# Rolling the middle of an unrolled mixture-of-experts stage into hardware loops, on one Trainium2 core

## The chip, the cores and the metric

The kernel runs on one core of a Trainium2 chip. The metric is the device time of one execution in microseconds. A core has five instruction streams that meet only at semaphores: TensorE (PE: matmuls, with its weight loads listed as PEld), VectorE (DVE), ScalarE (ACT), GpSimd (POOL) and SyncE (SP), which here issues the DMAs. Each engine reads its own program. Where the program is straight, every instruction is executed once; where it has a loop, the engine jumps back to code that it has had before and wait values are computed from the loop's counter. A difference within 0.2% of the time can't be told from no change.

## What is computed

Three layers in float32, on 4 x 576 = 2304 tokens of width 512.

```
# attention through 32 packed queries for each of 4 x 8 heads
p_packed = softmax(p k^T / 8) v            # 32 x 64
x = softmax(q p_packed^T / 8) p_packed     # 576 x 64, heads put side by side: 2304 x 512

# 8 experts, dense, weights from 8 Sinkhorn steps on exp(x @ w_gate)
out = 0
for e in range(8):
    h = maximum(x @ w1[e], 0)              # 2304 x 1024
    out += P[:, e:e+1] * (h @ w2[e])       # 2304 x 512

# MLP
r = maximum(out @ w_in, 0)                 # 2304 x 2048
result = (s * r * r + b) @ w_out
```

## The kernel before

Every float32 factor is split in two parts, hi and lo, and a product is three matmul passes (hi hi, hi lo, lo hi), in `three_passes`. The time has three stages. Attention comes first, with the order of its work written out by hand for each engine. The experts come next, from about 90 to 1310 us, and the MLP last.

**Groups.** The hidden units of the experts are worked in groups of 256 (`FG`), four groups to an expert (`PER_EXPERT`), 32 groups in all (`MOE_GROUPS`). Groups 0 to 4 are done plainly. Groups 5 (`SEVEN`) to 31 use a scheme with seven products in place of eight: since x is a product of small attention weights `a` and packed values, `x @ w1` is done as `a @ g`, where `g` (the packed values times w1) is a small matrix made for each group, and the 2 x 2 block product `a @ g` of one batch is done with seven block products and some sums.

**One group on each engine** goes in four steps (`UNITS7`), one for each batch of tokens:
- PE: `unit_of_seven`, seven products of three passes with 288 columns, into four PSUM banks; then `outputs`, four or five token tiles of `h @ w2` of 128 x 512, six matmuls each, into two PSUM banks in turn; after the first of these tiles `fill`, four matmuls of 256 columns toward `g` of a later group. Before tile t PE waits for `acc_done`, that is for DVE to have read tile t - 2's bank. Inside a unit PE waits for `p1_copied` (ACT has copied the first product) and twice for `joined` (DVE has made the sums U2 and U3), because the banks of those sums are written again.
- ACT: `unit_of_seven`, the copy of the first product, then two ReLUs that write `h_hi`; and `shift_fill`, eight small copies that place `g` in `g_raw`.
- DVE: `joins`, seven additions; then `output` for each tile, which waits for `y_full` and adds the tile times the token's gate to `acc`; and two `lo_of_joined`, which write `h_lo`. U2 and U3 are the first two additions.
- POOL: `split_heads` and `split_w2` split the weights that have been loaded into hi and lo; `blocks_of_batch`, once for each batch, makes the seven blocks of the next group's `g`.
- SP: loads the weights of each group, in a loop over the experts, four groups to a turn (`with sp.Fori(1, E) as e`).

All engines run groups 5 to 31 from straight code: PE, ACT and POOL through `groups_of_seven`, DVE through a loop of its own over `group_of_seven`, which is given the operation that adds a tile (`shared(e)`, with the column of the gate that belongs to expert e).

**The MLP** is 8 groups of 256 hidden units in five chunks of tokens each (`mlp_steps`). The first two groups are straight code, and the other six are a loop on PE, ACT and DVE, three turns of two groups:

```
with eng.Fori(1, MLP_GROUPS // 2) as mp:
    for par in range(2):
        for c in range(MC):
            step(mp * 2 + par, par, c)
```

POOL has a loop of the same three turns. In such a loop a wait such as `pe.wait_ge(acc_done, m * TILES + ...)` compares with a value that the engine makes from the counter with a register instruction.

Of the kernel before, what the change touches and what calls it, by code (L numbers as in the profile page):

```python
# [10 lines left out]
ds = bass.ds  # L11
# [7 lines left out]
def attention_moe_mlp(nc, q, k, v, p, w_gate, w1, w2, w_in, w_out, s_, b_, out):  # L19
# [3 lines left out]
    E, FE = w1.shape[0], w1.shape[2]  # L23
# [24 lines left out]
    PER_EXPERT = FE // FG  # L48
    MOE_GROUPS, MLP_GROUPS = E * PER_EXPERT, FM // FG
# [6 lines left out]
    with ExitStack() as ctx:  # L56
# [3 lines left out]
        def sb(name, shape, dt=F32, scope=ctx):  # L60
            return scope.enter_context(nc.sbuf_tensor(name, shape, dt))
# [15 lines left out]
        gate = sb("gate", [P, TILES, E])  # L77
# [222 lines left out]
        SEVEN = FIRST  # L300
# [21 lines left out]
        def hidden_count(g, b, f):  # L322
            return g * GC + (b * FC + f)

        def groups_of_seven(eng, group):
            for g in range(SEVEN, MOE_GROUPS):
                group(g, g % 2)

# [1 line left out]
        MCHUNKS = [(at, min(BANK, N - at)) for at in range(0, N, BANK)]  # L331
        MC = len(MCHUNKS)
        assert MC % 2 == 1 and all(n % P == 0 for _, n in MCHUNKS)

        def slot_of(par, c):
# [59 lines left out]
        def pieces_of_tile(t):  # L395
            found = []
            for b in range(B):
                for c, (_, n) in enumerate(CHUNKS):
                    for r in range(2):
                        at = first_col(b, c) + r * n  # L400
                        lo, hi = max(at, t * P), min(at + n, (t + 1) * P)
                        if lo < hi:
                            found.append((b, c, r, lo - at, hi - at, lo - t * P))
            return found
# [7 lines left out]
        def scores2_of(b, c):  # L412
            at = s2_bank(b, c) * BANK + BANK - H * NPACK
            _, rows, groups = PARTS[c]
            return PS[0:rows, at:at + groups * NPACK].rearrange("s (h n) -> s h n", n=NPACK)
# [176 lines left out]
        def _(pool):  # L592
# [157 lines left out]
            def group_of_seven(g, par):  # L750
# [5 lines left out]
                if ahead:  # L756
# [8 lines left out]
                    blocks_of_batch(g + 1, 1 - par, 3)  # L765

            groups_of_seven(pool, group_of_seven)
            split_in(MOE_GROUPS + 1, 1)
            pool.wait_ge(y_full, MOE_GROUPS * TILES)
# [10 lines left out]
        def _(act):  # L780
# [268 lines left out]
            for j in range(2):  # L1049
                shift_fill(SEVEN + 1, 0, j)  # L1050
            groups_of_seven(act, group_of_seven)

            def turned(some):
# [29 lines left out]
        def _(dve):  # L1083
# [138 lines left out]
            def output(g, tile, add):  # L1222
                dve.wait_ge(y_full, g * TILES + (tile + 1))
                add(acc[:, tile, :], bank(YB + tile % 2), tile).then_inc(acc_done, 1)
# [6 lines left out]

            def shared(e):
                def add(dst, y, tile):
                    share = gate[:, tile, e:e + 1]
                    return nc.vector.scalar_tensor_tensor(out=dst, in0=y, scalar=share, in1=dst,  # L1235
                                                          op0=ALU.mult, op1=ALU.add)
                return add
# [163 lines left out]
            def unit_and_tiles(g, b, g_out, tiles, add, between=None):  # L1401
                joins(g, b)
                for n, t in enumerate(tiles):
                    output(g_out, t, add)
                    if n < FC:
                        lo_of_joined(g, b, 1 - n)
                    if between:
                        between(t)

            def group_of_seven(g, add, between=None):  # L1410
                last = isinstance(g, int) and g == MOE_GROUPS - 1
                for n, (u, half, t0, t1) in enumerate(UNITS7):
                    of = 1 if n >= 2 else 0
                    tiles = range(of * UT + t0, of * UT + t1)
                    if n == 3 and last:
                        for t in tiles:
                            output(g, t, add)
                            between(t)
                    else:
                        unit_and_tiles(g + 1 if n == 3 else g, 2 * u + half, g, tiles, add, between if n >= 2 else None)  # L1420
# [8 lines left out]
            expert_group(UNSCALED, scaled_then_shared, ahead_of_seven)  # L1429
            for n in range(1, PER_EXPERT):  # L1430
                group_of_seven(UNSCALED + n, shared(1))
            for g in range(SEVEN + PER_EXPERT - 1, MOE_GROUPS - 1):
                group_of_seven(g, shared(g // PER_EXPERT))

            def inputs_lo(step):
# [51 lines left out]
        def _(pe):  # L1488
# [511 lines left out]

            eight_to_seven(SEVEN - 1, 0)
            groups_of_seven(pe, group_of_seven)

            def mlp_hidden(m, par, c, f):
# [61 lines left out]
```

## Time and profile before

| | |
|---|---|
| median of 3 runs | 1712.21 us (1711.3 to 1714.53) |
| profiled execution | 1711.3 us; its span 1709.5 us |
| PE busy | 1700.5 us |
| DVE, POOL, ACT busy | 1195.6, 1029.8 and 734.9 us |
| mean granted TensorE clock | 1.0 of full speed |
| instructions | 27307 |

The span is from the first to the last instruction of the profiled execution; the time has 1.8 us more around it. Busy shares are means over stages with different limits, so the views of a stretch say more than the page. Register, branch and semaphore instructions aren't shown in the views; they are part of the count of instructions. Instructions themselves are fetched by DMA, and the profile lists the packets of that as queues of the kind "instruction": q8 carries packets of 16 KB for PE, q14 packets of 8 KB for the others.

### The profile page before, as it was taken

Reading aid. Unit: us, or ns where it says so; the run is one execution under the profiler, and the core shown is the slowest. Engines: PE = TensorE matmul, PEld = TensorE weight load, DVE = VectorE, ACT = ScalarE, POOL = GpSimd, SP = SyncE. Lnnn points to the kernel's source line nnn. Section 1 sums busy time; section 2 is a strip of 40 time slices with the busy share of each in tenths; the row PEclk is TensorE's granted clock in tenths of the full one; section 3 lists DMA queues with packets and bytes.
Section 4 is the critical chain, followed back from the end, with each engine's and each line's share of the span. In section 5 each row is a group of like instructions: output and inputs, shape, how many; then the busy total and the mean of one; then the engine's idle time right before and its main releaser. Section 6 shows DMA issues by size and latency. Waiting matters only on the chain.

```text
span 1709.5 us, 27307 instructions
## 1 busy us (share of the span) xinstructions
PE 1700.5 (99%) x9933; PEld 1474.6 (86%) x9933; DVE 1195.6 (70%) x2119; ACT 734.9 (43%) x1672; POOL 1029.8 (60%) x1200
## 2 busy tenths in 40 slices
PE   9999999999999999999999999999999999999999
PEld 7888888888888888888888888888888888888887
DVE  4846646787777777787778787878787555555555
ACT  5644466454545444544445444545433222222222
POOL 1266669988888888788888877888872010111100
PEclk9999999999999999999999999999999999999999
DMA  9431111111112211111121111112101000000003
GB/s 281 122 81 38 50 38 25 38 49 39 38 38 51 49 38 38 50 38 38 38 62 38 38 43 45 38 38 48 40 25 38 13 20 18 25 25 25 0 0 110
DMA packets 71847, 79.71 MB, mean 47 GB/s; under 512 B 7984, under 2 KB 59184, under 8 KB 71728
## 3 DMA queue, kind: packets, MB, share of 16 engines
q1 hardware_dynamic: 71728, 78.15, 17.1%
q8 instruction: 72, 1.18, 0.3%
q14 instruction: 47, 0.39, 0.1%
HBM read 73.42 MB, written 4.72 MB: 46 GB/s over the span
## 4 chain that ended last, share of the span: by engine, by line
PE 96%; POOL 2%; ACT 1%; DMA 0%; issue 0%; DVE 0%; SPq 0%; POOLq 0%; DVEq 0%
PE PS L1490 94%; PE PS L1510 2%; ACT g_raw L782 1%; PE PS L1724 0%; DMA k_raw<-k_dram 0%; POOL w_lo L606 0%; POOL span_late L695 0%; POOL recombined L679 0%; POOL sums_of_a L687 0%; POOL w_lo L621 0%; POOL w_hi L604 0%; POOL span_late L697 0%; POOL a_parts L699 0%; ACT acc L812 0%; POOL g_slots L727 0%
## 5 line engine op out<-in xcount | busy, mean ns | idle before, releaser
L1490 PE MATMUL PS<-w_hi,h_hi 128*128 128x512 f32 x1440 | 564.6, 392 | 0.6 <-DVE acc L1235 0.6
L1490 PE MATMUL PS<-w_lo,h_hi 128*128 128x512 f32 x1440 | 563.1, 391 | 0.0
L1490 PE MATMUL PS<-w_hi,h_lo 128*128 128x512 f32 x1440 | 560.4, 389 | 0.0
L1235 DVE SCALAR_TENSOR_TENSOR acc<-PS,gate,acc 128x512 f32<-128x512 f32 x504 | 378.4, 751 | 178.9 <-PE PS L1490 178.9
L782 ACT ACTIVATE g_raw<-PS 32x256 f32<-32x256 f32 x992 | 372.0, 375 | 12.3 <-PE PS L1490 0.4
L1490 PEld LDWEIGHTS PS<-w_hi,h_lo 128*128 128x128 f32 x1440 | 270.5, 188 | 58.3
L1490 PEld LDWEIGHTS PS<-w_hi,h_hi 128*128 128x128 f32 x1440 | 270.8, 188 | 50.5 <-DVE acc L1235 0.8
L1490 PEld LDWEIGHTS PS<-w_lo,h_hi 128*128 128x128 f32 x1440 | 270.9, 188 | 46.9
L998 ACT ACTIVATE h_hi<-PS 128x576 fp32r<-128x576 f32 x216 | 128.9, 649 | 303.5 <-DVE PS L1371 303.5
L1490 PE MATMUL PS<-a_parts,g_slots 128*128 128x288 f32 x1296 | 225.1, 295 | 0.1
L604 POOL CAST w_hi<-stage 128x1024 fp32r<-128x1024 f32 (+1 forms) x78 | 76.6, 982 | 238.9 <-PE PS L1490 218.1
L1490 PEld LDWEIGHTS PS<-a_parts,g_slots 128*128 128x128 f32 x1296 | 195.7, 188 | 9.6 <-POOL g_slots L727 0.5
L1371 DVE TENSOR_TENSOR PS<-PS,snaps 128x288 f32<-128x288 f32 x432 | 177.3, 456 | 0.1
L1371 DVE TENSOR_TENSOR snaps<-PS,snaps 128x288 f32<-128x288 f32 x324 | 148.4, 458 | 38.7 <-ACT snaps L782 15.5
L606 POOL TENSOR_TENSOR w_lo<-stage,w_hi 128x1024 fp32r<-128x1024 f32 (+1 forms) x78 | 170.0, 2179 | 6.2
L1490 PE MATMUL PS<-sums_of_a,g_slots 128*128 128x288 f32 x972 | 164.1, 295 | 0.6 <-ACT snaps L782 0.6
L1230 DVE TENSOR_TENSOR acc<-PS,acc 128x512 f32<-128x512 f32 x180 | 124.2, 690 | 56.8 <-PE PS L1490 55.6
L1394 DVE SCALAR_TENSOR_TENSOR h_lo<-PS,h_hi 128x576 fp32r<-128x576 f32 x216 | 161.6, 748 | 0.0
L727 POOL TENSOR_TENSOR g_slots<-g_sums,g_slots 128x512 fp32r<-128x512 f32 x108 | 139.8, 1295 | 8.5
L1490 PEld LDWEIGHTS PS<-sums_of_a,g_slots 128*128 128x128 f32 x972 | 140.7, 188 | 0.8 <-ACT snaps L782 0.8
L782 ACT ACTIVATE snaps<-PS 128x288 f32<-128x288 f32 x108 | 44.4, 411 | 221.4 <-PE PS L1490 221.4
L1067 ACT ACTIVATE mlp_f<-PS 128x512 f32<-128x512 f32 (+1 forms) x80 | 44.4, 556 | 220.0 <-PE PS L1490 220.0
(158 smaller groups left out, 2155.8 us busy)
## 6 DMA issues: line engine op xcount, KB each, us to landing
stage<-moe_w_dram SPq DMA_DIRECT2D x96, 512.0 KB, 4.9
k_raw<-k_dram SPq DMA_DIRECT2D x8, 512.0 KB, 6.4
q_raw<-q_dram SPq DMA_DIRECT2D x8, 512.0 KB, 5.2
v_raw<-v_dram SPq DMA_DIRECT2D x8, 512.0 KB, 6.8
stage<-moe_w_in_dram SPq DMA_DIRECT2D x16, 256.0 KB, 3.0
stage<-moe_w_out_dram SPq DMA_DIRECT2D x8, 512.0 KB, 3.6
out_dram<-acc SPq DMA_DIRECT2D x16, 256.0 KB, 2.3
p_twice<-p_dram SPq DMA_DIRECT2D x8, 64.0 KB, 4.2
```

Source lines behind the costliest of these rows:

```text
L604: nc.gpsimd.tensor_copy(hi, src).then_inc(w1_ready, 1)
L606: nc.gpsimd.tensor_tensor(lo, src, hi.bitcast(F32), ALU.subtract).then_inc(w1_ready, 1)
L727: nc.gpsimd.tensor_tensor(lo[:, GS1:BLOCKS, :], g_sums[:], hi[:, GS1:BLOCKS, :].bitcast(F32), ALU.subtract).then_inc(g_split, 1)
L782: return nc.scalar.activation(dst, src, ACT.Copy)
L998: nc.scalar.activation(h_hi[:, f, b % 2 * S:(b % 2 + 1) * S].rearrange("p (i n) -> p i n", i=2), bank(HB + 2 * f, 2 * BANK).rearrange("p ( ...
L1067: nc.scalar.activation(mlp_f[:, slot, f, 0:n], bank(HB + 2 * slot + f, n), ACT.Relu).then_inc(relu_ready, 1)
L1230: return nc.vector.tensor_tensor(dst, y, dst, ALU.add)
L1235: return nc.vector.scalar_tensor_tensor(out=dst, in0=y, scalar=share, in1=dst, op0=ALU.mult, op1=ALU.add)
L1371: nc.vector.tensor_tensor(dst, bank(at, SPAN), term, ALU.add).then_inc(joined, 1)
L1394: nc.vector.scalar_tensor_tensor(out=h_lo[:, f, cols].rearrange("p (i n) -> p i n", i=2), in0=bank(HB + 2 * f, 2 * BANK).rearrange("p (i n ...
L1490: return nc.tensor.matmul(dst, lhsT, rhs, start=start, stop=stop)
L1510: last = nc.tensor.transpose(bank(unit_bank(unit))[0:m_, c0:c0 + k_], src, ident[0:k_, 0:k_])
```

## The change

`groups_of_seven`, which PE, ACT and POOL use, did groups 5 to 31 in straight code. It now does groups 5 to 28 in a loop of 12 turns with two groups each, and 29 to 31 in straight code. DVE did groups 5 to 30 in straight code ahead of a last, special one. It still does groups 5 to 7 so; groups 8 to 27 are a loop over experts 2 to 6, with four groups to a turn; 28 to 30 are straight again. For the loop, the gate's column is taken with `ds(e, 1)`, an offset that may come from a register.

```
         def groups_of_seven(eng, group):
-            for g in range(SEVEN, MOE_GROUPS):
+            with eng.Fori((SEVEN + 1) // 2, MOE_GROUPS // 2 - 1) as gp:
+                group(gp * 2 - 1, 1)
+                group(gp * 2, 0)
+            for g in range(MOE_GROUPS - 3, MOE_GROUPS):
                 group(g, g % 2)
...
             def shared(e):
                 def add(dst, y, tile):
-                    share = gate[:, tile, e:e + 1]
+                    share = gate[:, tile, ds(e, 1)]
...
             for n in range(1, PER_EXPERT):
                 group_of_seven(UNSCALED + n, shared(1))
-            for g in range(SEVEN + PER_EXPERT - 1, MOE_GROUPS - 1):
-                group_of_seven(g, shared(g // PER_EXPERT))
+            with dve.Fori(2, E - 1) as e:
+                for n in range(PER_EXPERT):
+                    group_of_seven(e * PER_EXPERT + n, shared(e))
+            for n in range(PER_EXPERT - 1):
+                group_of_seven(MOE_GROUPS - PER_EXPERT + n, shared(E - 1))
```

## Rows read from the trace of the kernel before

**Rows 1.** The page: span, busy time of each engine, granted clock.
```profile
span 1709.5 us, 27307 instructions
...
PE 1700.5 (99%) x9933; PEld 1474.6 (86%) x9933; DVE 1195.6 (70%) x2119; ACT 734.9 (43%) x1672; POOL 1029.8 (60%) x1200
...
PEclk9999999999999999999999999999999999999999
```

**Rows 2.** Windows, two in the expert stage, one in the MLP.
```profile
core 0: us, PE busy (x) PEld busy (x) DVE busy (x) ACT busy (x) POOL busy (x), PEclk, DMA share, GB/s
292.00:692.00 400.00, 399.45 (x2202) 352.30 (x2201) 317.71 (x574) 192.12 (x465) 332.02 (x412) 1.00 0.17 42
692.00:1092.00 400.00, 400.00 (x2204) 353.04 (x2203) 318.23 (x572) 194.62 (x472) 328.01 (x408) 1.00 0.18 43
...
1505.00:1603.00 98.00, 98.00 (x457) 82.10 (x456) 52.89 (x76) 24.58 (x40) 15.08 (x13) 1.00 0.07 21
```

**Rows 3.** The chain that ended last: start us, us, what.
```profile
539.26 754.45 PE PS L1490 x4153
```

**Rows 4.** Groups of DVE instructions on the page: busy us, mean ns, idle before.
```profile
L1235 DVE SCALAR_TENSOR_TENSOR acc<-PS,gate,acc 128x512 f32<-128x512 f32 x504 | 378.4, 751 | 178.9 <-PE PS L1490 178.9
...
L1371 DVE TENSOR_TENSOR snaps<-PS,snaps 128x288 f32<-128x288 f32 x324 | 148.4, 458 | 38.7 <-ACT snaps L782 15.5
```

**Rows 5.** Waits in 692 to 1092 us: us in total, times, longest.
```profile
ACT h_hi L998 <- DVE PS L1371: 121.1, 43, 3.0
...
DVE acc L1235 <- PE PS L1490: 67.2, 148, 0.6
POOL g_slots L715 <- ACT g_raw L782: 37.9, 10, 4.1
...
PEld PS L1490 <- DVE snaps L1371: 0.2, 1, 0.2
```

**Rows 6.** Timeline of DVE, last output of a step and the joins of the next.
```profile
801.13 0.75 DVE L1235 SCALAR_TENSOR_TENSOR acc<-PS,gate,acc 128x512 f32<-128x512 f32 x1 [0.61 <-PE PS L1490]
802.03 1.02 DVE L1371 TENSOR_TENSOR snaps<-PS,snaps 128x288 f32<-128x288 f32 x2 [0.15 <-ACT snaps L782]
...
803.89 1.18 DVE L1371 TENSOR_TENSOR PS<-PS,snaps 128x288 f32<-128x288 f32 x3
```

**Rows 7.** Timeline of PE's weight loads in the same unit.
```profile
802.39 0.45 PEld L1490 LDWEIGHTS PS<-sums_of_a,g_slots 128*128 128x128 f32 x3
802.78 0.86 PEld L1490 LDWEIGHTS PS<-a_parts,g_slots 128*128 128x128 f32 x6
803.59 0.19 PEld L1490 LDWEIGHTS PS<-w_hi,h_hi 128*128 128x128 f32 x1
```

**Rows 8.** Instruction fetches in 692 to 1092 us: packets, MB, share.
```profile
q8 instruction: 17, 0.28, 0.3%
q14 instruction: 13, 0.11, 0.1%
```

**Rows 9.** All DMA queues in 1505 to 1603 us, the MLP loop's second turn.
```profile
DMA packets 1632, 2.10 MB, mean 21 GB/s; under 512 B 96, under 2 KB 1120, under 8 KB 1632
...
q1 hardware_dynamic: 1632, 2.10, 6.7%
```

**Rows 10.** Instruction fetches in 1407 to 1505 us, the MLP loop's first turn.
```profile
q8 instruction: 4, 0.07, 0.3%
q14 instruction: 1, 0.01, 0.0%
```

**Rows 11.** DMA issues on the page: count, KB each, median us to landing.
```profile
stage<-moe_w_in_dram SPq DMA_DIRECT2D x16, 256.0 KB, 3.0
...
out_dram<-acc SPq DMA_DIRECT2D x8, 64.0 KB, 1.7
...
s_and_b<-moe_b_dram SPq DMA_DIRECT2D x1, 0.5 KB, 8.2
```

## The prediction

> **What bounds the kernel now.** I read the page first: the span is 1709.5 us, PE is busy for 1700.5 us of it, and the granted clock is at full speed throughout (the 2.4 GHz level) [rows 1]. So nearly all of the time is matmul time. Next I read the windows of the stage that the change rewrites (the groups of seven products, about 292 to 1294 us): PE is busy 399.45 and 400.00 us of two windows of 400 us [rows 2]. The chain that ended last agrees: one unbroken piece of 754.45 us with 4153 matmuls [rows 3]. By the code a group has 18 output tiles x 6, 28 products x 3 and 4 fills x 4 = 208 matmuls, so 4153 are 20 groups of 37.7 us. The reader should take two things from this. There is nothing to win in this stage: PE never stops, and the change removes no matmul. And there is no reserve: what stops PE once is added to the end.
>
> Behind PE stand engines that are fairly full. In the second window DVE is busy 318 of 400 us, POOL 328, ACT 195 [rows 2]. By the table of waits DVE idles 67.2 us there before outputs, waiting for PE, ACT 121.1 us for DVE, POOL 37.9 us for ACT's copies; PE's weight loads waited 0.2 us for a DVE join, once [rows 5]. This last row is small but telling: the join is the place where PE nearly touches DVE. The timeline shows how nearly. DVE starts its last output at 801.13, takes 0.75, and starts the first join of the next unit at 802.03 [rows 6]. A join takes 0.46 us [rows 4], so the first is done at 802.49. The product that needs it has its first weight load at 802.78 [rows 7]: 0.29 us to spare. The second join ends at 803.05 (802.03 + 1.02 for two); the product that needs it is three loads behind 802.78, at about 803.19 (6 loads end at 803.64): 0.14 us to spare.
>
> **The change part by part.** It removes no arithmetic, transfer or wait. It rolls 24 of 27 groups into a loop of 12 turns of two groups on PE, ACT and POOL, and 20 groups into a loop of 5 turns of four groups on DVE. It adds three things.
>
> 1. *Wait values.* Every wait in a loop compares with a value made from the counter, so a register instruction stands ahead of each distinct value. Counted from the code, a group has about 43 such values on PE, 54 on DVE, 17 on ACT, 33 on POOL. Cost: the kernel's last stage is such a loop already (two blocks of 256 hidden units a turn). There PE is busy 98.00 of 98.00 us, with a back edge inside the window [rows 2]. So on PE the values and the branch cost nothing that shows: they run under queued matmuls (0.23 us each there, 0.13 us each for the narrow products). On DVE an output takes 0.75 us and its values are made under the instruction before it. Where two joins follow each other in 0.37 us (three take 1.18 us [rows 6]) one or two values must fit; no row prices one, so I bound it: 0 below; above, if every one of 24 x 4 units lost 0.1 us beyond the 0.14 to spare, +10 us. I take 0.
>
> 2. *The gate's column* becomes a register address in 360 outputs. PE needs the result of a tile two tiles later. A tile is 6 x 0.227 = 1.36 us, an output 0.75 us, and DVE idles 0.45 to 0.61 us before most of them (67.2/148, and 0.61 in the timeline) [rows 5, 6]. Address work ahead of the wait is hidden by that idle time; if the cover were gone, a delay beyond about 0.2 us (two tiles less an output and the hand-over both ways) in each output would add its excess 360 times. No row shows one; I take 0.
>
> 3. *The jump back.* Instructions are fetched by DMA: 17 packets of 16 KB on PE's queue and 13 of 8 KB on the other engines' queue in 400 us of straight code [rows 8]. PE's queue brings 0.28 MB for 4407 matmuls and loads, some 64 bytes for each. In the last stage the first turn fetches 4 and 1 packets [rows 10], the second none at all [rows 9]: the loop was still on chip. PE's body there is 912 loads and matmuls (456 each); the new one is 832 (2 x 208 x 2), with a like number of values, so it should stay on chip too: 11 back edges at 0, and some 36 fetches fewer, worth 0 because PE was not waiting for them. ACT's new body is 88 operations and about 34 values, near the largest that rows show resident on these engines: DVE's in the last stage, 76 operations and about 57 values, 133. POOL's is 76 operations, some 38 separate waits and 66 values, about 180; should it miss, the first work after its jump is a weight split, and POOL has an idle piece of some 4 us (37.9/10 = 3.8 each) further on in that group, so I cost it at 0.
>
> DVE is different. Four groups are 4 x (54 operations + 12 separate waits + 54 values) = 480 instructions before any address work, up to 550 with it, some 31 to 35 KB: almost four times what rows show resident there. I take it that the head of the loop is gone when DVE jumps to it, at 4 back edges (5 turns). Rows can't show this; a page can: the Trainium skill, "Runtime: NRT & Kernel Launch", section "Instruction fetch mechanics", gives 32 KiB (512 instructions) for most engines and 128 KiB for PE, and says that a taken branch to code outside waits for a fetch. By that page the miss is sure for 550 and nearly so for 480, since the next block is fetched ahead.
>
> Price of a miss: a read from memory that nothing was asked early for. Nearest rows, issue to landing: 1.7 us (64 KB stores), 3.0 us (256 KB loads), 8.2 us (a 0.5 KB load behind others) [rows 11]. I take 3.0. The branch is read right after the last output is handed over, 801.13 in the window shown; code arrives at 804.1; I allow 0.3 us for branch and first values (an estimate that no row carries; 0 to 0.75 is possible), and the join is done 0.46 us later, at 804.9. PE wants it at 802.78, so it stops for 2.1 us. PE has no idle time to catch up in, so this stays: 4 x 2.1 = 8.5 us. With 1.7 us it is 4 x 0.8 = 3.2 us; with 8.2 us, 4 x 7.3 = 29 us. Late after it: nothing new, since all engines wait on PE and DVE together.
>
> **Sum.** The profiled execution took 1711.3 us (1709.5 + 1.8 around it), 0.9 under the median of 1712.2. 1711.3 + 8.5 = 1719.8, on the median's footing 1720.7.
>
> **Rivals.**
> *A. Nothing happens* (DVE's loop stays on chip, or the fetch is short enough). For it: the last stage's loops are free. Against it: the body is 3.6 times theirs. Time 1712.2, up to 1715.6. Chance 0.24.
> *B. Every unit pays*: register work on the join chain exceeds 0.14 us, or the register address lengthens each output. For it: margins of 0.14 and 0.29 us. Against it: PE's 98.00 of 98.00 us, with waits of the same kind on DVE, though not so tight. At 0.1 us a unit, 96 units, +10 us; at 0.2 us, +19 us: 1722 to 1731. Chance 0.12.
> *C. PE's own loop misses.* The Trainium skill, "Advanced Engine Details and Errata", section "ISA Cache", says "Only 2 cache lines!" of 256 instructions each. Taken for PE, that would have made the last stage's loop fetch in each turn; the trace disagrees: no packet in 1505 to 1603 [rows 9]. Worked out as a mechanism of this kernel: 11 back edges x 3.0 us less about 0.8 us of queued matmuls = +24 us, 1736. Chance 0.03.
> *D. Faster.* Fewer fetches leave the weight transfers and PE's prefetch alone. It would have to take from the 0.55 us that PE idled in 292 to 692, and the whole kernel has 9.0 us of PE idle time, nearly all outside this stage [rows 1, 2]. Best case 1711.6; over 0.2% it would need 3.4 us that the stage doesn't have. Chance 0.03.
> *Forecast: DVE misses at its 4 back edges.* Chance 0.58; its own range 1715.4 to 1725.
>
> **How the numbers follow.** Differences within 0.2% (3.4 us) can't be told from no change. Slower: 0.58 less the 0.02 in which the fetch is as short as 1.7 us, plus B and C: 0.71. Same: 0.24 + 0.02 = 0.26. Faster: 0.03. The range must take in part of A, because it is the second likeliest, so it begins at 1712.0; above it goes to 1730, through most of B and a fetch of about 6 us. Outside it lie C, the dearest fetches and a quarter of A.
>
> **What would show it.** In the new profile PE should be busy without a gap except at four places 151 us apart (4 x 37.7), each a wait of PE for a DVE join of about 2 us. Instruction packets: PE's queue should fall from 72 to about 36 over the run, with none from the loop's second turn to its end; the other queue should carry 4 or 5 packets in every 151 us, DVE's body again and again. If the matmuls of each unit have a gap, B is right. If the four gaps are there and shorter than 1 us, my price was wrong. If gaps come every 75 us, it is PE's, ACT's or POOL's loop. If DVE's packets stop after the first turn, its memory is larger than I think, and the forecast is wrong.

## The result and the profile after

The changed kernel takes 1733.6 us (median of 4 runs, 1730.98 to 1736.25) against 1712.7 us before: ratio 1.0121, 95% interval 1.0103 to 1.0140, so 20.7 us slower. The forecast was 1720.7 us, in a range from 1712.0 to 1730.

The page of the profiled execution, with the rows that answer to [rows 1], and its instruction queues:

```profile
span 1729.4 us, 30251 instructions
...
PE 1707.5 (99%) x9933; PEld 1479.4 (86%) x9933; DVE 1195.0 (69%) x2119; ACT 736.4 (43%) x1672; POOL 1030.3 (60%) x1200
...
q8 instruction: 36, 0.59, 0.1%
q14 instruction: 43, 0.35, 0.1%
```

The span is 19.9 us longer with the same matmuls. It splits in two: PE stands idle for 1729.4 - 1707.5 = 21.9 us where it was 9.0, which is +12.9; and PE is busy for 7.0 us more with the same work. By their place, the first is stalls, and most of the second is a slower PE; the exact shares come below. 2944 instructions more are executed (register and branch instructions: the counts of work are the same), and no engine's busy time shows them. PE's packets fell from 72 to 36.

The stalls, in the table of waits (us in total, times, longest):

```profile
DVE snaps L1375 <- issue: 16.0, 4, 4.0
PEld PS L1497 <- DVE snaps L1375: 14.2, 4, 3.6
PE PS L1497 <- DVE snaps L1375: 13.3, 4, 3.4
```

There are four, as many as DVE's loop has back edges, and all are PE waiting for DVE's first join (13.3 us by the matmuls, 14.2 by their weight loads). DVE in its turn waited for "issue", that is for nothing that the profile shows. Before, in 400 us of this stage, PE's loads had waited once, 0.2 us, for this join [rows 5]. The timeline of the second stall (DVE's rows, then PE's):

```profile
713.29 0.75 DVE L1239 SCALAR_TENSOR_TENSOR acc<-PS,gate,acc 128x512 f32<-128x512 f32 x1 [0.61 <-PE PS L1497]
718.08 0.95 DVE L1375 TENSOR_TENSOR snaps<-PS,snaps 128x288 f32<-128x288 f32 x2 [4.04 <-issue]
...
718.59 1.16 PE L1497 MATMUL PS<-a_parts,g_slots 128*128 128x288 f32 x6 [3.36 <-DVE snaps L1375]
...
719.67 1.19 DVE L1375 TENSOR_TENSOR PS<-PS,snaps 128x288 f32<-128x288 f32 x3
```

The join starts 4.79 us after the last output began; before it was 0.90 us [rows 6]. DVE is 3.9 us late, and PE, with 0.3 us to spare, about 3.6. The joins themselves are no slower: from the first to the last three it is 1.59 us, where it was 1.86.

The trace has more of this jump than its views show. DVE's branch is executed at 713.37, under the last output, and its next instruction at 717.86, 4.49 us later; at the four jumps back it is 4.4 to 4.5 us. Between the two one instruction packet of 8 KB moves, from 715.64 to 716.26. So the packet itself takes 0.62 us; 2.3 us pass before it starts and 1.6 us after it has ended.

The slower PE shows in windows around the first two stalls, and just behind the third and the fourth (columns as in [rows 2]):

```profile
558.00:563.00 5.00, 1.73 (x13) 1.44 (x12) 1.01 (x4) 0.09 (x1) 4.25 (x8) 1.00 0.34 65
563.00:566.50 3.50, 3.50 (x13) 2.91 (x12) 1.77 (x5) 1.20 (x2) 2.92 (x4) 0.54 0.00 0
...
714.00:719.00 5.00, 1.64 (x13) 1.41 (x11) 0.93 (x4) 0.09 (x1) 4.25 (x8) 1.00 0.37 71
719.00:722.50 3.50, 3.50 (x20) 3.01 (x20) 3.10 (x8) 1.95 (x5) 2.92 (x4) 1.00 0.00 0
...
873.90:877.40 3.50, 3.50 (x12) 2.94 (x11) 1.72 (x6) 1.20 (x2) 2.92 (x4) 0.51 0.00 0
1030.90:1034.40 3.50, 3.50 (x12) 2.88 (x11) 2.02 (x4) 2.25 (x5) 3.00 (x3) 0.51 0.00 0
```

The first two stretches of 3.5 us just behind a stall are counted busy throughout, but in the first PE starts 13 matmuls at a granted clock of 0.54, in the second 20 at 1.00. Behind the first stall PE ran at the 1.2 GHz level. The third and the fourth look like the first, so that happened behind three of the four stalls.

Both traces have the same 9933 matmuls, so each can be compared with itself, by its start. The four stalls and what follows each put the next matmuls back by 5.2, 3.7, 5.3 and 5.3 us: 19.4 of the 19.9 us. The second, with no fall of the clock, gives the price of a stall alone, 3.7 us; the fall adds about 1.5 us. In all that is some 14.9 us for the stalls and 4.5 us for the clock. The split by busy and idle time (12.9 and 7.0) is coarser, since the ends of matmuls are modelled and part of each stall is counted as busy.

The instruction packets of one turn of DVE's loop, 562.5 to 718.5 us:

```profile
DMA packets 5317, 6.33 MB, mean 41 GB/s; under 512 B 192, under 2 KB 4288, under 8 KB 5312
q1 hardware_dynamic: 5312, 6.29, 16.3%
q14 instruction: 5, 0.04, 0.1%
```

PE's queue carries nothing in the loop. The other queue carries 5 packets of 8 KB, a body of DVE's size, again in each turn. Their times show which blocks they are. They start at 593.77, 634.43, 678.08 and, behind the next jump, at 715.63 and 718.48. Between the first three DVE executes 127 and 130 instructions by the trace, so a packet starts each time DVE enters a block of about 128 instructions, and brings the next block. The body (468 instructions by the trace) lies in four blocks: entering the second, third and fourth brought the third, the fourth and, at 678.08, a fifth that DVE never gets to before it jumps. The head is the one that then has to be fetched on demand.

### The profile page after: what moved, and what is told of

Read it like the earlier page. It is cut to its first block, busy times and chain, and to the rows that moved or that the text cites. A ratio compares the mean times of both kernels' runs of the same rounds, so it can differ in the third digit from the quotient of the medians.

```text
span 1729.4 us, 30251 instructions
## 1 busy us (share of the span) xinstructions
PE 1707.5 (99%) x9933; PEld 1479.4 (86%) x9933; DVE 1195.0 (69%) x2119; ACT 736.4 (43%) x1672; POOL 1030.3 (60%) x1200
## 4 chain that ended last, share of the span: by engine, by line
PE 94%; POOL 2%; issue 1%; ACT 1%; DMA 1%; DVE 0%; SPq 0%; DVEq 0%; POOLq 0%; ACTq 0%
PE PS L1497 92%; PE PS L1517 2%; ACT g_raw L786 1%; DMA stage<-moe_w_dram 0%; PE PS L1731 0%; POOL w_lo L610 0%; DMA k_raw<-k_dram 0%; POOL span_late L699 0%; POOL w_hi L608 0%; POOL recombined L683 0%; POOL sums_of_a L691 0%; POOL w_lo L625 0%; DVE snaps L1375 0%; POOL span_late L701 0%; POOL a_parts L703 0%
## 5 line engine op out<-in xcount | busy, mean ns | idle before, releaser
L1497 PE MATMUL PS<-a_parts,g_slots 128*128 128x288 f32 x1296 | 225.8, 296 | 13.5 <-DVE snaps L1375 13.3
L1497 PEld LDWEIGHTS PS<-a_parts,g_slots 128*128 128x128 f32 x1296 | 195.8, 188 | 23.7 <-DVE snaps L1375 14.2
```

The costliest lines, as they stand in the source:

```text
L1497: return nc.tensor.matmul(dst, lhsT, rhs, start=start, stop=stop)
```

## The experiments

All comparisons of time are with the kernel before, measured beside each; the edits are shown against the changed kernel.

**DVE's loop alone.** `groups_of_seven` is straight again:

```
-            with eng.Fori((SEVEN + 1) // 2, MOE_GROUPS // 2 - 1) as gp:
-                group(gp * 2 - 1, 1)
-                group(gp * 2, 0)
-            for g in range(MOE_GROUPS - 3, MOE_GROUPS):
+            for g in range(SEVEN, MOE_GROUPS):
                 group(g, g % 2)
```

> Only DVE's loop (groups 8 to 27, four to a turn) is kept; PE, ACT and POOL run straight code as before. Theory F (fetch): DVE's jump back goes to code that is no longer on chip, at 4 back edges; each stops PE for about 3.4 us, and after three of four PE's clock fell to half for 3.4 us. Then this kernel loses as much as the whole change: +17 to +22 us against the kernel before, four PE waits for the DVE join. Rival R (the loops of PE, ACT and POOL, or their register work, carry a part): less than +15 us.

Measured: 1733.3 us, ratio 1.0124 (1.0108 to 1.0141), +21 us. Its waits show the same four:

```profile
DVE snaps L1372 <- issue: 15.2, 4, 3.9
...
PE PS L1494 <- DVE snaps L1372: 12.5, 4, 3.2
```

DVE's loop carries the whole loss. The clock fell behind three of the four here too, but the first fall lasted 6.8 us in place of 3.4 and the fourth stall had none.

**The loops of PE, ACT and POOL alone.** DVE is straight again:

```
-            with dve.Fori(2, E - 1) as e:
-                for n in range(PER_EXPERT):
-                    group_of_seven(e * PER_EXPERT + n, shared(e))
+            for g in range(2 * PER_EXPERT, (E - 1) * PER_EXPERT):
+                group_of_seven(g, shared(g // PER_EXPERT))
```

> Only the loops of PE, ACT and POOL are kept (12 turns of two groups); DVE runs straight code. Theory F: these bodies stay on chip and their 11 back edges and register values lie under queued work, so the time is that of the kernel before within 3 us, and no PE wait over 1 us in the expert stage. Rival R: +3 us or more, with gaps of PE every 75 us.

Measured: 1712.5 us, ratio 1.0003 (0.9991 to 1.0015). Eleven back edges on three engines cost nothing, and PE's 36 packets fewer bring nothing.

**A smaller DVE body.** The whole change, but DVE's loop is two loops:

```
             with dve.Fori(2, E - 1) as e:
-                for n in range(PER_EXPERT):
-                    group_of_seven(e * PER_EXPERT + n, shared(e))
+                with dve.Fori(0, PER_EXPERT // 2) as half:
+                    for n in range(2):
+                        group_of_seven(e * PER_EXPERT + half * 2 + n, shared(e))
```

> The whole change, but DVE's four groups to a turn become an inner loop of two turns with two groups each. DVE jumps more often (5 inner and 4 outer back edges), has the same register values, the same gate column from a register, but a body of about 234 instructions in place of 468. Theory F: body and head stay on chip, no stall: within 3 us of the kernel before. Rival V (register values or the register address of the gate slow the joins or the outputs): the loss stays, +15 us or more. Rival J (a jump back costs 4 us in itself): 9 jumps, more than +35 us.

Measured: 1711.7 us, ratio 1.0002 (0.9992 to 1.0011). In the trace DVE's next instruction follows each jump back after 0.3 us, where it was 4.4 us and more in the changed kernel. Rivals V and J fall: the register values, the gate's address and more jumps than in the changed kernel are all there, and the loss is not. The page:

```profile
span 1709.0 us, 30371 instructions
...
q14 instruction: 21, 0.17, 0.0%
```

**The same DVE body with a prefetch hint.**

```
-            with dve.Fori(2, E - 1) as e:
+            with nc.Fori(2, E - 1, engines=[dve.engine], hint_back_edge=True) as e:
```

 Theory F: the stalls go, within 3 us of the kernel before, at the price of the same number of fetches or more. Rivals V and J: the loss stays at +20 us.

Measured: 1716.0 us, ratio 1.0026 (1.0016 to 1.0035): 4.5 us above the kernel before by the ratio, 16 us below the changed one, and outside the 3 us that I had given. The four stalls are gone. One that I had not expected stands behind the loop:

```profile
1171.75 0.46 DVE L1375 TENSOR_TENSOR snaps<-PS,snaps 128x288 f32<-128x288 f32 x1 [0.15 <-ACT snaps L786]
1174.92 0.46 DVE L1375 TENSOR_TENSOR snaps<-PS,snaps 128x288 f32<-128x288 f32 x1 [2.72 <-issue]
```

The last output of the loop begins at 1160.73 and the next 15 operations run as ever; then DVE stands for 2.7 us inside straight code, between two joins. In the last turn the hint was wrong: the branch falls through, and what fits is that a block behind the loop was not asked for in time: an instruction packet starts at 1173.21, inside this stall. The stall puts PE back by 2.5 us; the rest of the 4.5 us isn't explained. I also had the packets wrong: 23 on that queue, where the changed kernel has 43. In a whole turn, 562.5 to 713 us, the only queue with packets is that of the data:

```profile
DMA packets 5312, 6.29 MB, mean 42 GB/s; under 512 B 192, under 2 KB 4288, under 8 KB 5312
...
q1 hardware_dynamic: 5312, 6.29, 16.8%
```

So the body of four groups was on chip in full. What drove its head out in the changed kernel is shown by the first turn, before any jump. From the start of the span to 478.5 us the queue of the other engines has 15 packets in both traces, and the pairs start within 1.4 us of each other. Then DVE enters the last block of the body, and the queues in 515 to 530 us are, first in the changed kernel, then with the hint:

```profile
q1 hardware_dynamic: 1056, 1.05, 31.6%
q14 instruction: 1, 0.01, 0.2%
```

```profile
q1 hardware_dynamic: 1056, 1.05, 31.6%
```

That one packet, at 522.18, is the next block in straight order, which isn't executed before the jump; the jump at 557.37 then misses. With the hint it isn't fetched, and the jump hits. This makes the 5 packets of a turn: the four blocks of the body, and that one.

**Fewer jumps.** Two turns of eight groups in place of five of four, about 930 instructions a turn:

```
-            with dve.Fori(2, E - 1) as e:
-                for n in range(PER_EXPERT):
-                    group_of_seven(e * PER_EXPERT + n, shared(e))
+            with dve.Fori(1, E // 2 - 1) as ep:
+                for i in range(2):
+                    for n in range(PER_EXPERT):
+                        group_of_seven(ep * (2 * PER_EXPERT) + i * PER_EXPERT + n, shared(ep * 2 + i))
+            for n in range(PER_EXPERT):
+                group_of_seven((E - 2) * PER_EXPERT + n, shared(E - 2))
```

> The whole change, but DVE's loop has 2 turns of eight groups (about 930 instructions) in place of 5 turns of four: one back edge in place of four. Theory F: one stall of PE of 3.4 us and one possible fall of the clock (up to 1.7 us more): +3.5 to +5.5 us against the kernel before. A rival in which the loss comes with the looped groups and not with the jumps: 16 of 20 groups are still looped, +16 us.

Measured: 1717.5 us, ratio 1.0024 (1.0014 to 1.0034), +4.1 us. One stall:

```profile
DVE snaps L1375 <- issue: 4.3, 1, 4.3
...
PE PS L1500 <- DVE snaps L1375: 3.6, 1, 3.6
```

The loss goes with the jumps that miss, not with the looped groups.

**The same body at two places.** Three groups to a turn (338 instructions by the trace) and six turns; between the two kernels only the slot of a 128-slot block at which the loop begins differs, 0 (shown) or 100. In both, the loop scales by expert 2's column throughout, which gives another result for the same work.

```
-            with dve.Fori(2, E - 1) as e:
-                for n in range(PER_EXPERT):
-                    group_of_seven(e * PER_EXPERT + n, shared(e))
+            with nc.Fori(0, 6, engines=[dve.engine], head_slot={dve.engine: 0}) as t:
+                for n in range(3):
+                    group_of_seven(t * 3 + 2 * PER_EXPERT + n, shared(2))
+            for g in range(2 * PER_EXPERT + 18, (E - 1) * PER_EXPERT):
+                group_of_seven(g, shared(E - 2))
```

> The whole change, but DVE's loop has three groups to a turn (about 351 instructions, 6 turns, groups 8 to 25), its head placed on the first slot of a fetch block of 128, so that the body touches 3 blocks. In the loop every tile is scaled by the gate column of expert 2 (the output is not the reference's), which changes no work. Theory F with an on-chip memory of four blocks, of which one is taken by the block fetched ahead: 3 + 1 fit, the head is still there, no stall: within 3 us of the kernel before. If the limit is lower than that: 5 stalls, about +22 us.

> As the kernel of three groups to a turn with its head at slot 0, but the head at slot 100 of its block: 100 + 351 = 451 slots, so the same body touches 4 blocks. Also here the loop uses the gate column of expert 2 throughout. Theory F with four blocks, one of them for the block ahead: the head is gone, 5 stalls of PE of 3.4 us and some falls of the clock, +17 to +27 us. If only the length of the body counts: as with slot 0.

Measured: at slot 0 1712.3 us, ratio 0.9995 (0.9986 to 1.0005); at slot 100 1740.2 us, ratio 1.0160 (1.0143 to 1.0177). The page of the first, and page and waits of the second:

```profile
span 1710.9 us, 30072 instructions
...
q14 instruction: 24, 0.20, 0.0%
```

```profile
span 1734.9 us, 30072 instructions
...
q14 instruction: 50, 0.41, 0.1%
...
DVE snaps L1375 <- issue: 20.8, 5, 4.3
...
PE PS L1499 <- DVE snaps L1375: 17.4, 5, 3.6
```

The same 30072 instructions are executed in both. Placed over three blocks the body stays on chip; placed over four it misses at every jump, five times (DVE's next instruction 4.3 to 4.7 us after the jump, against 0.3 to 0.4 at slot 0).

**PE kept busy in the stall.** With DVE's loop alone, at groups 12, 16, 20 and 24:

```
+                if b == 1 and isinstance(g, int) and g in (12, 16, 20, 24):
+                    pe.wait_ge(acc_done, g * TILES - 1)
+                    for n in range(24):
+                        mm(bank(YB, SPAN), g_blocks[b][:, 0, G22, :], t4[0][0] if isinstance(t4[0], list) else t4[0], True, True)
                 pe.wait_ge(joined, of_unit(g, b, U2))
```

> DVE's loop only, as in the first experiment, and 24 more matmuls of 288 columns on PE (3.2 us) at the four places where DVE's jump stops it, just ahead of the wait for the join; they write a PSUM bank that is free there and change no result. They lie inside the stall. If the clock falls because PE stood idle in the stall, it now stays at full speed throughout, PE's wait shrinks to about 0.3 us, and the time is 13.6 to 15 us above the kernel before: 3 to 7 us less than with DVE's loop only. If the fall of the clock has another cause, nothing is gained.

Measured: 1728.0 us, ratio 1.0083 (1.0066 to 1.0100), +14.2 us; by the ratios 7.0 us less than with DVE's loop alone, though the ends of the intervals leave 1 to 13. The profile is sharper. Windows of 7.5 us around the three stalls behind which the clock fell with DVE's loop alone, first of this kernel, then of the one with DVE's loop alone:

```profile
558.00:565.50 7.50, 7.29 (x51) 6.83 (x50) 3.05 (x8) 0.41 (x1) 6.66 (x10) 1.00 0.40 79
713.00:720.50 7.50, 6.84 (x49) 6.42 (x48) 2.92 (x7) 0.41 (x1) 6.43 (x9) 1.00 0.35 71
868.00:875.50 7.50, 7.50 (x54) 7.21 (x53) 3.50 (x9) 1.13 (x3) 6.44 (x9) 1.00 0.33 67
```

```profile
557.00:564.50 7.50, 4.25 (x20) 3.73 (x19) 2.85 (x8) 0.75 (x3) 6.45 (x10) 0.74 0.23 45
714.00:721.50 7.50, 4.60 (x21) 4.04 (x20) 2.93 (x8) 1.11 (x3) 6.45 (x10) 0.77 0.21 39
869.00:876.50 7.50, 4.34 (x23) 3.67 (x23) 3.12 (x8) 1.25 (x3) 6.45 (x10) 0.88 0.26 51
```

DVE is as late in both (its "issue" wait is 16.2 and 15.2 us in all), but with matmuls in the stall the clock stays at 1.00. PE's idle wait for the join, 12.5 us in all, is 0.9. So the fall of the clock is a second price of the stall, and it needs PE to stand idle; idle time alone doesn't explain it, since one stall of four had no fall.

**PE's loop twice as long.** DVE straight, ACT and POOL in turns of two groups, PE in six turns of four:

```
+            if eng is nc.tensor:
+                with eng.Fori(1, (MOE_GROUPS - 4) // 4) as gp:
+                    for n in range(4):
+                        group(gp * 4 + n + 1, (n + 1) % 2)
+            else:
...
```

> DVE runs straight code, ACT and POOL keep their loops of two groups, and PE's loop has four groups to a turn (6 turns, some 1840 instructions in blocks of 256, so it touches 8 or 9 blocks; the loop of two touches 4 or 5). Theory F: PE's on-chip memory holds a number of blocks too. If that is eight, as the Trainium skill's page Runtime: NRT & Kernel Launch gives it (128 KiB, section Instruction fetch mechanics), the head is gone at 5 back edges; each costs a fetch of about 4 us less about 1 us of queued matmuls, and the clock may fall after it: +14 to +28 us. Rival: PE runs far enough ahead, or holds more: within 3 us of the kernel before.

Measured: 1749.2 us, ratio 1.0215 (1.0198 to 1.0232), +36.8 us, or 7.4 us for a jump: above the range I gave. Waits and PE's queue:

```profile
q8 instruction: 84, 1.38, 0.3%
...
PE PS L1501 <- issue: 27.1, 5, 5.7
```

PE stands for 5.4 us on the mean at each of five jumps even after it has used up its queued matmuls, and the mean clock of the run is 0.991. Matmul by matmul, each jump puts PE back by 6.9 to 8.3 us. The form is DVE's: at the first jump (branch at 440.3) a packet of its queue starts at 444.9 and a second at 448.2, when PE has just gone on. So PE misses too, and its miss is dearer. How many blocks PE's memory holds isn't shown by this one size.

**POOL's loop with a miss in it.** DVE straight, POOL in six turns of four groups with the head at slot 100:

```
+            if eng is nc.gpsimd:
+                with nc.Fori(1, (MOE_GROUPS - 4) // 4, engines=[eng.engine], head_slot={eng.engine: 100}) as gp:
+                    for n in range(4):
+                        group(gp * 4 + n + 1, (n + 1) % 2)
+            else:
...
```

> DVE runs straight code, PE and ACT keep their loops of two groups, and POOL's loop has four groups to a turn (6 turns, about 344 instructions) with its head at slot 100 of a block, so that it touches four blocks, as the DVE loop that stalled five times. Theory F: POOL misses at 5 back edges and stands for about 4 us, but its work there has about 4 us of reserve, so PE sees little: within 3 us of the kernel before, while the other engines' queue carries some 20 packets more than with loops of two groups. If a miss costs on any engine: +15 us or more.

Measured: 1711.7 us, ratio 0.9996 (0.9987 to 1.0006). POOL did miss, five times, with 57 packets on the queue against 30 in the kernel with loops of two groups:

```profile
q14 instruction: 57, 0.47, 0.1%
...
POOL w_hi L613 <- issue: 15.4, 5, 3.2
...
POOL g_slots L724 <- ACT g_raw L791: 71.5, 24, 7.2
```

It stood 15.4 us, and 11 us of that came off its wait for ACT's copies, which in the kernel with loops of two groups was:

```profile
POOL g_slots L719 <- ACT g_raw L786: 82.6, 24, 7.2
```

Here the miss cost nothing, because POOL had the reserve for it.

## Why the prediction was wrong

Mechanism, place and count of the stalls were right. The price of one was too low, and what the clock takes behind it was missing.

- *Nothing to win in the stage*: right. No kernel here is faster than the one before.
- *Wait values at 0, gate address at 0*: right; the smaller DVE body has both and costs nothing. Rival B is out.
- *PE, ACT and POOL at 0*: right (1.0003), PE's fetches fell to 36 as said, and POOL's reserve does hide a miss.
- *DVE misses at 4 back edges, PE waits at the first join*: right. The Trainium skill's rule ("Runtime: NRT & Kernel Launch", "Instruction fetch mechanics"), 32 KiB for most engines, agrees with the two placements: three blocks of 8 KB plus one fetched ahead fit, four do not. Its block of 16 KiB and window of two pages don't describe DVE here: the packets are of 8 KB. The body itself fitted, as the hint showed. My count of 480 instructions was near (468), but I had rested the miss on the size of the body, with the block ahead in half a sentence; that block is the whole reason.
- *The price of a miss*: this term was mis-sized. I took 3.0 us for the code to arrive and 0.3 us for branch and values, so the join would start 3.3 us after the last output. It starts after 4.79 us: from the branch to the next instruction alone it is 4.49 us. A stall by itself puts PE back by 3.7 us in place of 2.1, which is 6.4 us of the error over four. The prices that I chose from were of data transfers, between 1.7 and 8.2 us, and none was of a fetch on demand.
- *"Late after it: nothing new"*: wrong, and missing from the sum altogether. After three of four stalls PE ran 3.4 us at half clock, about 1.5 us each, 4.5 us. With the 6.4 us this is 10.9 of the 11.4 us by which the profiled span (+19.9) exceeds the forecast (+8.5).
- *The range*: its upper end took in a dearer fetch, but no second price, and stopped 3.6 us short.

What isn't settled is why the clock did not fall after the second stall, which was as long as the others; and why a packet that takes 0.62 us starts 2.3 us after the branch and is followed by 1.6 us more.

## What to carry to other kernels

Rolling straight code into a loop was free here as long as the body stayed on chip, and its register work hid behind queued instructions. On DVE, once the body plus the block fetched ahead no longer fitted, each jump cost a fetch on demand: count instructions with their wait values, and mind at which slot the head falls. The cost lands where the jump is, so ask what reserve the engine has just there; split the loop, or put the jump on an engine or at a place with slack. When a stall is priced on a PE that was never idle, add what the clock may take afterwards (1.5 us behind three of four stalls here).

## What the runs showed that I had not expected

- A fetch on demand made DVE 3.9 us late; PE's own, in the kernel with the longer PE loop, held it 5.4 us beyond its queued work. DVE's packet takes 0.62 us of the 4.49 from the branch to the next instruction.
- The block that pushes the loop's head out is the one behind the loop, fetched ahead at the end of each turn and not executed before the jump. In the first turn it is one packet, at 522.18 us, that the hinted kernel doesn't have.
- Stalls of PE of about 3.5 us were followed by a stretch at the 1.2 GHz level in three of four cases in the changed kernel; matmuls in the stall kept the clock at 1.00.
- The same instructions cost 0 or 28 us by the slot at which the loop began (1712.3 and 1740.2 us).
- A hint for the jump back removed four stalls and left one of 2.7 us at the loop's exit, and cut the packets from 43 to 23, none of them in the loop's turns.
